# Scores and state product of a decayed linear attention in eight 64 x 32 array tiles, causal quarters only

## The chip, the cores and the metric

The kernel runs on one core of one Trainium2 chip. The metric is the device time of one execution in microseconds. TensorE (PE) multiplies, VectorE (DVE) and ScalarE (ACT) work element by element, GpSimd (POOL) does a little arithmetic on single columns, and SyncE (SP) issues the transfers.

## The reference, cut to what matters

```python
# q, k, v, f_logit: (4, 8, 768, 48)
f = 1.0 / (1.0 + np.exp(-f_logit))
for t in range(S):
    state = f[:, :, t, :, None] * state + np.einsum('bhd,bhe->bhde', k[:, :, t], v[:, :, t])
    y[:, :, t] = np.einsum('bhd,bhde->bhe', q[:, :, t], state)
# y as rows (3072, 384); RMS norm with weights rms_g; d_ff 1536
x = (silu(xn @ w_gate) * (xn @ w_val)) @ w_out
# d_ff 2048; g is 0 below -1, h above 1, (h + 1)^2 / 4 between
y = g(x @ w_in) @ w_out
```

## The kernel before, in words

The sequence is cut into chunks of C = 128 positions; there are 24 (six for each of four batches), three to a tile of N = 384 rows, so NT = 8 tiles. The heads lie in pairs: NP = 4 pairs p, and the heads r = 0, 1 of a pair occupy partitions 0 to 47 and 64 to 111 (HP = 64, D = 48). For a chunk, VectorE makes two cumulative products of the decays by scans (`after`, and `qd` by way of L721), the decayed keys `kd` and queries `qd`, and the decayed state `decayed`. TensorE then

- turns kd into kdT by four transposes (turn_kd, L300), which ScalarE copies out of the accumulator ta;
- multiplies keys by queries (score, L314): for each pair one matmul of head 0 into bank tb and one of head 1 into bank ta, each of 64 rows by 128 columns of the array with 128 moving columns. VectorE multiplies both by the 0/1 matrix `causal` (mask_scores, L752), which clears the keys that come after a query;
- computes the state's update k^T v (update, L324) into tb, which VectorE adds to `decayed` (update_state, L763);
- makes y (attend) in y_ps: for each pair the decayed state times qd in four tiles of 112 rows by 32 columns, for both heads at once (L338, 96 moving columns, of which the part between different heads is zero in `state`), and then scores times v for each head in four tiles of 128 by 32 (L344, 48 moving columns);
- turns the normalised rows (turn_x, L352), which become the input x of the projections, split in a high and a low part.

The plain float32 operands make each of these matmuls two passes in the trace. The projections of the two MLPs (L403, L425, L429, L467, L479, L483) run over the split high and low operands with 384 moving columns.

The order is written out by hand. Chunks 0 to 2 are made ahead of everything (first_attention), with matmuls between that only keep the array busy (L375). Then tile i goes through 12 steps j of the first MLP while the attention of tile i + 1 is put between the projections: 36 slots, three to a step, and chunk c of the tile is offset by 10 slots (WINDOW). On TensorE slot 4 is turn_kd, 6 score, 9 update and attend, 13 turn_x; each engine has its own list for the same slots. TensorE, VectorE and ScalarE run tiles 1 to 6 in a hardware loop (Fori). Tile 7 has no attention beside it. The second MLP follows.

Waits are semaphores that count chunks. y_made rises twice a chunk, after each half of the pairs; it frees v_sb, qd, kd and decayed. turn_kd writes into ta as soon as the masks of the chunk before are done. normalise (L769) reads y_ps when POOL has made rstd (L286, L289), and raises xs_ready. When decays are too small a general path after the main block repeats everything; it doesn't run with these inputs.

Of the kernel before, what the change touches and what calls it, by code (L numbers as in the profile page):

```python
# [17 lines left out]
F32 = mybir.dt.float32  # L18
# [40 lines left out]
def build(nc, qkf, v, rms_g, wb, wc, out, y_rows):  # L59
    ctx = ExitStack()  # L60
    with ctx:
# [29 lines left out]
        state = sb("state", [P, 2, NP, 2 * D])  # L91
        decayed = sb("decayed", [P, NP, 2 * D])
# [14 lines left out]
        causal = sb("causal", [P, C])  # L107
# [11 lines left out]
        y_ps = bank("y_ps")  # L119
        ta = bank("ta")  # L120
        tb = bank("tb")

# [80 lines left out]
        with nc.Block() as block:  # L203
# [3 lines left out]
            def _(sp):  # L207
# [23 lines left out]
                for n in range(1, CT):  # L231
                    sp.wait_ge(y_made, 2 * n)
                    load_v(n)
                    load_wb(n + 1)
# [5 lines left out]
                sp.wait_ge(y_made, 2 * CT)  # L240
# [6 lines left out]
                sp.wait_ge(y_made, 2 * CT + 2)  # L247
                load_v(CT + 1)
                load_wb(11)
                with sp.Fori(CT + 2, NCH) as n:  # L250
                    sp.wait_ge(qd_ready, n)
                    load_raw(n)
                    sp.wait_ge(y_made, n * 2)
                    load_v(n)
                stages = len(wc_stages)
                sp.wait_ge(qd_ready, NCH)
                for j in range(JC):
                    if j == 2:
                        sp.wait_ge(y_made, 2 * NCH)
# [14 lines left out]
            def _(pool):  # L274
                nc.gpsimd.memset(minus_half[:, :], -0.5).then_inc(consts_ready, 1)
                nc.gpsimd.memset(eps_col[:, :], EPS).then_inc(consts_ready, 1)
                nc.gpsimd.memset(causal[:, :], 1.0).then_inc(consts_ready, 1)
                nc.gpsimd.memset(ident[:, :], 0.0).then_inc(consts_ready, 1)
                pool.wait_ge(consts_ready, 4)
                nc.gpsimd.affine_select(out=causal[:, :], in_=causal[:, :], compare_op=ALU.is_ge, fill=0.0,  # L280
                                        base=0, pattern=[[1, C]], channel_multiplier=-1).then_inc(consts_ready, 1)
# [12 lines left out]
            def _(pe):  # L294
                def turn_kd(n, c):
                    pe.wait_ge(kd_ready, n + 1)
                    if not isinstance(n, int) or n > 0:
# [5 lines left out]
                def score(n, c, first=False):  # L303
# [7 lines left out]
                    for p in range(NP):  # L311
                        for r, t in enumerate((tb, ta)):
                            rows = slice(r * HP, (r + 1) * HP)
                            mm = pe.matmul(t[:, p * C:(p + 1) * C], kd[rows, c % 2, p, :], qd[rows, c % 2, p, :],  # L314
                                           start=True, stop=True)
                    mm.then_inc(scores_made, 1)

                def update(n):
# [3 lines left out]
                    for p in range(NP):  # L322
                        for r in range(2):
                            mm = pe.matmul(tb[r * HP:r * HP + D, p * D:(p + 1) * D], kdT[:, p, r * HP:r * HP + D],  # L324
                                           v_sb[:, r, p, :], start=True, stop=True)
                    mm.then_inc(update_made, 1)

                def attend(n, c, half):
                    if half == 0:
                        pe.wait_ge(scores_ready, n * 2 + 2)  # L330
                        pe.wait_ge(decayed_ready, n + 1)
                        if not isinstance(n, int) or n > 0:
                            pe.wait_ge(xs_ready, n)
                    for p in range(half * NP // 2, (half + 1) * NP // 2):
                        o = p * 2 * D
                        for s in range(C // QW):
                            q = slice(s * QW, (s + 1) * QW)
                            pe.matmul(y_ps[q, o:o + 2 * D], qd[0:PR, c % 2, p, q], decayed[0:PR, p, :],  # L338
                                      start=True, stop=False, skip_group_check=True)
# [15 lines left out]
                def attention(i, slot):  # L355

                    for c in range(CT):
# [884 lines left out]
```

## Time and profile before

| | us |
|---|---|
| median of 3 runs | 984.48 (984.31 to 984.51) |
| profiled execution | 984.23 |
| its span | 982.5 |
| PE matmuls busy | 966.8 (8227 records) |
| DVE busy | 585.9 (1196) |
| ACT busy | 341.8 (624) |
| POOL busy | 22.4 (58) |

The span runs from the first to the last instruction. Matmuls are pipelined: the duration of one is its latency, and the distance from one start to the next is what it costs. "PEld" is the loading of a matmul's stationary operand. Columns "128*32 128x48" are the part of the array (rows * columns) and the moving operand.

### The profile page before, as it was taken

How to read it: one execution, taken by the hardware profiler on the slowest of the kernel's cores; microseconds unless marked ns; L12 is line 12 of the kernel's file. 1: busy time of each engine (PE TensorE's matmuls, PEld its weight loads, DVE VectorE, ACT ScalarE, POOL GpSimd, SP SyncE). 2: the span in 40 equal slices, each digit the busy share in tenths (PEclk: the TensorE clock that was granted, in tenths of full speed). 3: DMA queues.
4: the chain of work that ended last, by engine and by line, in shares of the span. 5: the costliest groups of instructions: out<-in, count | busy, mean ns of one | idle time of the engine just before them, and what ended most of it. 6: DMA issues, size and time to landing. Idle time of an engine off the chain costs nothing.

```text
span 982.5 us, 20662 instructions
## 1 busy us (share of the span) xinstructions
PE 966.8 (98%) x8227; PEld 943.4 (96%) x8227; DVE 585.9 (60%) x1196; ACT 341.8 (35%) x624; POOL 22.4 (2%) x58
## 2 busy tenths in 40 slices
PE   6899999999999999999999999999999999999998
PEld 6899999999999999999999999999999999999998
DVE  8778665574674765665565565555545554545454
ACT  2343322322322222223224454344344344434433
POOL 0100000000000000000000000000000000000000
PEclk9999999999999999999999999999999999999999
DMA  5541111011120110111120400000000000000000
GB/s 194 190 149 43 40 42 50 32 48 40 40 71 9 61 52 13 68 40 40 40 87 17 136 27 1 25 0 24 0 24 0 24 0 19 5 5 19 0 25 25
DMA packets 15774, 42.32 MB, mean 43 GB/s; under 512 B 1408, under 2 KB 8064, under 8 KB 15744
## 3 DMA queue, kind: packets, MB, share of 16 engines
q1 hardware_dynamic: 15744, 41.88, 12.5%
q8 instruction: 23, 0.38, 0.2%
q14 instruction: 7, 0.06, 0.0%
HBM read 37.16 MB, written 4.72 MB: 43 GB/s over the span
## 4 chain that ended last, share of the span: by engine, by line
PE 95%; DVE 3%; issue 1%; POOL 0%; ACT 0%; DMA 0%; DVEq 0%; POOLq 0%
PE gate_ps L403 15%; PE val_ps L403 15%; PE acc L479 13%; PE gate_ps L467 10%; PE val_ps L467 10%; PE acc L425 10%; PE acc L483 7%; PE acc L429 5%; PE tb L314 2%; PE y_ps L338 2%; PE y_ps L344 2%; PE tb L324 1%; DVE qd L721 1%; PE ta L300 1%; DVE after L700 1%
## 5 line engine op out<-in xcount | busy, mean ns | idle before, releaser
L837 DVE TENSOR_TENSOR h_lo<-h_buf,h_hi 128x384 fp32r<-128x384 f32 x224 | 123.3, 551 | 13.2 <-ACT h_hi L648 6.2
L641 ACT ACTIVATE act_buf<-act_buf,half_col 128x384 f32<-128x384 f32 x128 | 78.8, 615 | 140.5 <-DVE act_buf L887 140.5
L479 PE MATMUL acc<-h_hi,w_hi 128*128 128x384 f32 x381 | 127.5, 335 | 0.0
L479 PE MATMUL acc<-h_hi,w_lo 128*128 128x384 f32 x381 | 127.4, 334 | 0.0
L584 ACT ACTIVATE act_buf<-gate_ps 128x384 f32<-128x384 f32 x96 | 47.2, 492 | 177.1 <-PE gate_ps L403 177.1
L589 ACT ACTIVATE h_hi<-h_buf 128x384 fp32r<-128x384 f32 x96 | 50.5, 526 | 167.6 <-DVE h_buf L832 167.6
L403 PE MATMUL gate_ps<-x_hi,w_hi 128*128 (+1 forms) x288 | 99.2, 344 | 1.0 <-issue 0.6
L425 PE MATMUL acc<-h_hi,w_hi 128*128 128x384 f32 x288 | 99.1, 344 | 0.0
L403 PE MATMUL val_ps<-x_hi,w_hi 128*128 (+1 forms) x288 | 99.1, 344 | 0.0
L403 PE MATMUL gate_ps<-x_hi,w_lo 128*128 (+1 forms) x288 | 96.5, 335 | 0.0
L403 PE MATMUL val_ps<-x_hi,w_lo 128*128 (+1 forms) x288 | 96.4, 335 | 0.0
L403 PE MATMUL gate_ps<-x_lo,w_hi 128*128 (+1 forms) x288 | 96.4, 335 | 0.0
L425 PE MATMUL acc<-h_hi,w_lo 128*128 128x384 f32 x288 | 96.4, 335 | 0.0
L403 PE MATMUL val_ps<-x_lo,w_hi 128*128 (+1 forms) x288 | 96.4, 335 | 0.0
L648 ACT ACTIVATE h_hi<-h_buf 128x384 fp32r<-128x384 f32 x128 | 67.2, 525 | 80.4 <-DVE h_buf L892 80.4
L483 PE MATMUL acc<-h_lo,w_hi 128*128 128x384 f32 x381 | 86.5, 334 | 0.0
L826 DVE TENSOR_TENSOR h_buf<-gate_ps,act_buf 128x384 f32<-128x384 f32 x96 | 53.1, 553 | 52.6 <-ACT act_buf L584 52.2
L832 DVE TENSOR_TENSOR h_buf<-val_ps,h_buf 128x384 f32<-128x384 f32 x96 | 53.5, 557 | 38.0 <-PE val_ps L403 36.2
L887 DVE TENSOR_SCALAR act_buf<-val_ps 128x384 f32<-128x384 f32 x64 | 35.6, 557 | 67.0 <-PE val_ps L467 67.0
L479 PEld LDWEIGHTS acc<-h_hi,w_hi 128*128 128x128 f32 x381 | 71.5, 188 | 0.6
L479 PEld LDWEIGHTS acc<-h_hi,w_lo 128*128 128x128 f32 x381 | 71.5, 188 | 0.0
L887 DVE TENSOR_SCALAR act_buf<-gate_ps 128x384 f32<-128x384 f32 x64 | 35.5, 555 | 55.3 <-PE gate_ps L467 55.3
(117 smaller groups left out, 1989.3 us busy)
## 6 DMA issues: line engine op xcount, KB each, us to landing
raw<-qkf_dram SPq DMA_DIRECT2D x21, 768.0 KB, 4.3
x<-wb_dram SPq DMA_DIRECT2D x12, 576.0 KB, 5.2
v_sb<-v_dram SPq DMA_DIRECT2D x24, 192.0 KB, 2.8
out_dram<-x SPq DMA_DIRECT2D x7, 576.0 KB, 2.8
raw<-wc_dram SPq DMA_DIRECT2D x7, 384.0 KB, 3.1
x<-qkf_dram SPq DMA_DIRECT2D x2, 768.0 KB, 6.8
kd<-wc_dram SPq DMA_DIRECT2D x3, 384.0 KB, 3.1
qd<-wc_dram SPq DMA_DIRECT2D x3, 384.0 KB, 3.9
```

Source lines behind the costliest of these rows:

```text
L403: mm = pe.matmul(bank[:, 0:N], wb_part(w, j, part, k), x[:, par, k, :], start=(k == 0 and x is x_hi and w is w_hi), stop=(k == KM - 1 and ...
L425: pe.matmul(acc[:, m, 0:N], wb_part(w, j, 2, m), h_hi[:, j % 2, :], start=(j == 0 and w is w_hi), stop=False)
L467: mm = pe.matmul(t[:, 0:N], wc_part(w, j, 0, k), x[:, i % 2, k, :], start=(k == 0 and x is x_hi and w is w_hi), stop=(k == KM - 1 and w is ...
L479: pe.matmul(acc[:, m, 0:N], wc_part(w, j, 1, m), h_hi[:, j % 2, :], start=(j == 0 and w is w_hi), stop=False)
L483: mm = pe.matmul(acc[:, m, 0:N], wc_part(w_hi, j, 1, m), h_lo[:, j % 2, :], start=False, stop=(j == JC - 1))
L589: nc.scalar.activation(h_hi[:, j % 2, :], h_buf[:, j % 2, :], ACT.Copy).then_inc(h_hi_ready, 1)
L641: nc.scalar.activation(act_buf[:, j % 2, :], act_buf[:, j % 2, :], ACT.Square, bias=half_col[:, :], scale=0.5).then_inc(square_ready, 1)
L648: nc.scalar.activation(h_hi[:, j % 2, :], h_buf[:, j % 2, :], ACT.Copy)\
L826: nc.vector.tensor_tensor(h_buf[:, j % 2, :], gate_ps[:, 0:N], act_buf[:, 0, :], ALU.mult)\
L832: nc.vector.tensor_tensor(h_buf[:, j % 2, :], val_ps[:, 0:N], h_buf[:, j % 2, :], ALU.mult)\
L837: nc.vector.tensor_tensor(h_lo[:, j % 2, :], h_buf[:, j % 2, :], h_hi[:, j % 2, :].bitcast(F32), ALU.subtract).then_inc(done, 1)
L887: nc.vector.tensor_scalar(act_buf[:, j % 2, :], t[:, 0:N], 1.0, -1.0, ALU.min, ALU.max)\
```

## The change

The score product is cut into quarters of 32 keys (QW). A quarter s of an even pair is multiplied only by the queries from 32 s on, so with 128, 96, 64 and 32 columns. In odd pairs the order of the four key quarters is reversed in kd, in v and in the mask, so their quarters have 32, 64, 96 and 128 columns. With the two heads that makes eight tiles of 64 rows by 32 columns. The three chunks of the opening use all 128 columns for every quarter. The product of the decayed state (recall) gets the same eight tiles, one head at a time with 48 columns, and stands ahead of update. y has a bank for each head, the second one shared with ta (in the opening: banks 1 and 2 of acc); columns of y, weights and rms_g are ordered by head parity. State and decayed lose their zero blocks. Update is cut at row 32 into two tiles for each head. turn_kd waits for xs_ready. y_made rises once a chunk. kd is made by two instructions. POOL makes the second mask. The loops over tiles 1 to 6 become straight code on TensorE, ScalarE and VectorE.

```diff
-        state = sb("state", [P, 2, NP, 2 * D])
-        decayed = sb("decayed", [P, NP, 2 * D])
+        state = sb("state", [P, 2, NP, D])
+        decayed = sb("decayed", [P, NP, D])
-        causal = sb("causal", [P, C])
+        causal = sb("causal", [P, 2, C])
-        y_ps = bank("y_ps")
-        ta = bank("ta")
+        y_ps = ctx.enter_context(nc.psum_tensor("y_ps", [P, 2, 512], F32))
         tb = bank("tb")
+        ta = y_ps[:, 1, :]
+        y_first = acc[:, 1:3, :]
...
+                for s in range(C // QW):
+                    rows = slice(s * QW, (s + 1) * QW)
+                    pool.wait_ge(consts_ready, 6 + s)
+                    nc.gpsimd.affine_select(out=causal[rows, 1, :], in_=causal[rows, 1, :], compare_op=ALU.is_ge,
+                                            fill=0.0, base=s * QW + QW - C, pattern=[[1, C]],
+                                            channel_multiplier=-1).then_inc(consts_ready, 1)
...
                 def turn_kd(n, c):
                     pe.wait_ge(kd_ready, n + 1)
-                    if not isinstance(n, int) or n > 0:
+                    if not isinstance(n, int) or n >= CT:
+                        pe.wait_ge(xs_ready, n)
+                    elif n > 0:
                         pe.wait_ge(scores_ready, 2 * n)
...
                     for p in range(NP):
-                        for r, t in enumerate((tb, ta)):
-                            rows = slice(r * HP, (r + 1) * HP)
-                            mm = pe.matmul(t[:, p * C:(p + 1) * C], kd[rows, c % 2, p, :], qd[rows, c % 2, p, :],
-                                           start=True, stop=True)
+                        for s in range(C // QW):
+                            t0 = 0 if first else C - (s + 1) * QW if p % 2 else s * QW
+                            for r, t in enumerate((tb, ta)):
+                                rows = slice(r * HP, (r + 1) * HP)
+                                mm = pe.matmul(t[s * QW:(s + 1) * QW, p * C + t0:(p + 1) * C],
+                                               kd[rows, c % 2, p, s * QW:(s + 1) * QW],
+                                               qd[rows, c % 2, p, t0:C], start=True, stop=True)
                     mm.then_inc(scores_made, 1)
+
+                def recall(n, c, y):
+                    pe.wait_ge(scores_ready, n * 2 + 2)
+                    pe.wait_ge(decayed_ready, n + 1)
+                    if not isinstance(n, int) or n > 0:
+                        pe.wait_ge(xs_ready, n)
+                    for p in range(NP):
+                        for s in range(C // QW):
+                            q = slice(s * QW, (s + 1) * QW)
+                            for r in range(2):
+                                rows = slice(r * HP, (r + 1) * HP)
+                                pe.matmul(y[q, r, p * D:(p + 1) * D], qd[rows, c % 2, p, q], decayed[rows, p, :],
+                                          start=(p == 0), stop=False, skip_group_check=True)
...
-                            mm = pe.matmul(tb[r * HP:r * HP + D, p * D:(p + 1) * D], kdT[:, p, r * HP:r * HP + D],
-                                           v_sb[:, r, p, :], start=True, stop=True)
+                            for d0, d1 in ((0, QW), (QW, D)):
+                                rows = slice(r * HP + d0, r * HP + d1)
+                                mm = pe.matmul(tb[rows, p * D:(p + 1) * D], kdT[:, p, rows],
+                                               v_sb[:, r, p, :], start=True, stop=True)
...
-                def attend(n, c, half):
...
+                def attend(n, y):
+                    for p in range(NP):
                         for r in range(2):
-                            h = slice(o + r * D, o + (r + 1) * D)
                             for s in range(C // QW):
                                 q = slice(s * QW, (s + 1) * QW)
-                                mm = pe.matmul(y_ps[q, h], scores[:, r, p, q], v_sb[:, r, p, :],
+                                mm = pe.matmul(y[q, r, p * D:(p + 1) * D], scores[:, r, p, q], v_sb[:, r, p, :],
                                                start=False, stop=True, skip_group_check=True)
...
                         elif o == 9:
+                            recall(n, c, y_ps)
                             update(n)
-                            attend(n, c, 0)
-                            attend(n, c, 1)
+                            attend(n, y_ps)
...
                     for n in range(CT):
+                        recall(n, n, y_first)
                         update(n)
-                        attend(n, n, 0)
+                        attend(n, y_first)
                         if n + 1 < CT:
                             turn_kd(n + 1, n + 1)
-                        attend(n, n, 1)
-                        if n + 1 < CT:
                             score(n + 1, n + 1, True)
...
-                with pe.Fori(1, NT - 1) as i:
+                for i in range(1, NT - 1):
                     gated_mlp(i, i + 1)
...
-                    nc.vector.tensor_tensor(kd[:, c % 2, :, :], raw[:, 1, :, :], after[:, :, :], ALU.mult)\
-                        .then_inc(kd_ready, 1)
+                    nc.vector.tensor_tensor(kd[:, c % 2, 0::2, :], raw[:, 1, 0::2, :], after[:, 0::2, :], ALU.mult)
+                    turned, k_odd, after_odd = (x.rearrange("d a (s t) -> d a s t", s=C // QW) for x in
+                                                (kd[:, c % 2, 1::2, :], raw[:, 1, 1::2, :], after[:, 1::2, :]))
+                    nc.vector.tensor_tensor(turned[:, :, ::-1, :], k_odd, after_odd, ALU.mult).then_inc(kd_ready, 1)
```

The loops of ScalarE and VectorE change as TensorE's does. The masks, the square sum and the normalisation read the new layouts with as many elements as before. v is turned on the host as well, and the general path gets a copy of v that isn't (`v_rows`).

## Rows read from the trace of the kernel before

**Rows 1.** Page, part 1: busy time, share of the span, instructions of each engine.
```profile
PE 966.8 (98%) x8227; PEld 943.4 (96%) x8227; DVE 585.9 (60%) x1196; ACT 341.8 (35%) x624; POOL 22.4 (2%) x58
```

**Rows 2.** Stretches: length, busy time of each engine, granted clock, DMA share, GB/s.
```profile
0.00:40.00 40.00, 29.72 (x520) 27.25 (x521) 30.89 (x74) 12.29 (x22) 5.60 (x16) 1.00 0.63 223
40.00:100.00 60.00, 58.33 (x663) 54.73 (x662) 48.35 (x94) 24.36 (x42) 2.25 (x6) 1.00 0.26 90
280.00:340.00 60.00, 60.00 (x669) 57.72 (x668) 36.69 (x85) 16.76 (x36) 2.43 (x6) 1.00 0.11 36
```

**Rows 3.** TensorE's waits: us in total, times, longest.
```profile
PE acc L429 <- DVE h_lo L837: 1.3, 2, 0.8
```

**Rows 4.** Timeline of a score product: start, us, engine, line, operation.
```profile
324.55 0.33 PE L403 MATMUL gate_ps<-x_lo,w_hi 128*128 x1
324.72 0.34 PE L403 MATMUL gate_ps<-x_hi,w_lo 128*128 x1
324.99 0.37 PE L314 MATMUL tb<-qd,kd 64*128 64x128 f32 x1
325.00 0.37 PE L314 MATMUL ta<-qd,kd 64*128 64x128 f32 x1
325.20 0.27 PE L314 MATMUL tb<-qd,kd 64*128 64x128 f32 x1
...
325.87 0.27 PE L314 MATMUL tb<-qd,kd 64*128 64x128 f32 x1
325.88 0.27 PE L314 MATMUL ta<-qd,kd 64*128 64x128 f32 x1
326.08 0.45 PE L403 MATMUL val_ps<-x_hi,w_hi 128*128 x1
```

**Rows 5.** Timeline of update and attend in slot 9.
```profile
301.53 0.56 PE L324 MATMUL tb<-v_sb,kdT 128*48 128x48 f32 x16
302.02 0.37 PE L338 MATMUL y_ps<-decayed,qd 112*32 112x96 f32 x8
302.21 0.36 PE L344 MATMUL y_ps<-v_sb,scores 128*32 128x48 f32 x16
302.39 0.35 PE L338 MATMUL y_ps<-decayed,qd 112*32 112x96 f32 x8
302.56 0.35 PE L344 MATMUL y_ps<-v_sb,scores 128*32 128x48 f32 x16
...
303.52 0.44 PE L403 MATMUL gate_ps<-x_hi,w_hi 128*128 x1
```

**Rows 6.** Timeline of the weight loads of one group.
```profile
302.02 0.16 PEld L338 LDWEIGHTS y_ps<-decayed,qd 112*32 112x32 f32 x8
```

**Rows 7.** Timeline of VectorE in the opening.
```profile
13.53 0.55 DVE L746 TENSOR_TENSOR decayed<-state,whole 128x384 f32<-128x384 f32 x1
13.99 0.69 DVE L730 TENSOR_TENSOR kd<-x,after 128x512 f32<-128x512 f32 x1
14.60 0.72 DVE L763 TENSOR_TENSOR state<-tb,decayed 48x192 f32<-48x192 f32 x2
```

**Rows 8.** Timeline of the engines around a tile's first turn_kd.
```profile
322.08 0.55 DVE L837 TENSOR_TENSOR h_lo<-h_buf,h_hi 128x384 fp32r<-128x384 f32 x1
322.42 0.34 PE L425 MATMUL acc<-h_hi,w_lo 128*128 128x384 f32 x1
322.69 0.45 PE L429 MATMUL acc<-h_lo,w_hi 128*128 128x384 f32 x1
```

**Rows 9.** The chain that ended last, in the opening: start, us, what.
```profile
23.00 0.53 PE ta L300 x4
```

**Rows 10.** DMA queues: 0 to 100 us (first row) and 166 to 520 us (others).
```profile
q8 instruction: 9, 0.15, 0.6%
...
DMA packets 6816, 15.93 MB, mean 45 GB/s; under 512 B 544, under 2 KB 4384, under 8 KB 6816
q1 hardware_dynamic: 6816, 15.93, 13.7%
```

More of the change, by code:

```diff
@@ L56, with build @@
 SMALLEST = 2.0 ** -60
-def build(nc, qkf, v, rms_g, wb, wc, out, y_rows):
+def build(nc, qkf, v, v_rows, rms_g, wb, wc, out, y_rows):
     ctx = ExitStack()
@@ L231, in _ @@
                 for n in range(1, CT):
-                    sp.wait_ge(y_made, 2 * n)
+                    sp.wait_ge(y_made, n)
                     load_v(n)
@@ L239, in _ @@
                     load_wb(j)
-                sp.wait_ge(y_made, 2 * CT)
+                sp.wait_ge(y_made, CT)
                 load_v(CT)
@@ L246, in _ @@
                 load_wb(10)
-                sp.wait_ge(y_made, 2 * CT + 2)
+                sp.wait_ge(y_made, CT + 1)
                 load_v(CT + 1)
@@ L252, in _ @@
                     load_raw(n)
-                    sp.wait_ge(y_made, n * 2)
+                    sp.wait_ge(y_made, n)
                     load_v(n)
@@ L258, in _ @@
                     if j == 2:
-                        sp.wait_ge(y_made, 2 * NCH)
+                        sp.wait_ge(y_made, NCH)
                     if j >= stages:
@@ L374, in keep_warm @@
                     for _ in range(count):
-                        pe.matmul(acc[:, 0, 0:P], ident[:, :], causal[:, :], start=True, stop=True)
+                        pe.matmul(acc[:, 0, 0:P], ident[:, :], causal[:, 0, :], start=True, stop=True)
                 def first_attention():
@@ L682, in _ @@
                 gated_mlp(0, 1, split=True)
-                with act.Fori(1, NT - 1) as i:
+                for i in range(1, NT - 1):
                     gated_mlp(i, i + 1)
@@ L740, in decay_state @@
                     if not isinstance(n, int) or n > 0:
-                        dve.wait_ge(y_made, n * 2)
+                        dve.wait_ge(y_made, n)
                     if c > 0:
@@ L761, in update_state, with normalise @@
                     for r in range(2):
-                        rows, cols = slice(r * HP, r * HP + D), slice(r * D, (r + 1) * D)
-                        ins = nc.vector.tensor_tensor(state[rows, 1, :, cols], u[rows, :, :],
-                                                      decayed[rows, :, cols], ALU.add)
+                        rows = slice(r * HP, r * HP + D)
+                        ins = nc.vector.tensor_tensor(state[rows, 1, :, :], u[rows, :, :],
+                                                      decayed[rows, :, :], ALU.add)
                     ins.then_inc(state_ready, 1)
-                def normalise(n):
+                def normalise(n, y=y_ps):
                     dve.wait_ge(rstd_ready, n + 1)
-                    nc.vector.scalar_tensor_tensor(out=xs[:, :], in0=y_ps[:, 0:DM], scalar=rstd[:, :],
-                                                   in1=g_rows[:, :], op0=ALU.mult, op1=ALU.mult)\
+                    heads = [x[:, :].rearrange("t (r m) -> t r m", r=2) for x in (xs, g_rows)]
+                    nc.vector.scalar_tensor_tensor(out=heads[0], in0=y[:, :, 0:NP * D], scalar=rstd[:, :],
+                                                   in1=heads[1], op0=ALU.mult, op1=ALU.mult)\
                         .then_inc(xs_ready, 1)
@@ L935, in _ @@
                         dve.wait_ge(g_loaded, 16)
-                    normalise(n)
+                    normalise(n, y_first)
                 rest_x(0, CT - 1, (gate_ps, val_ps)[(CT - 1) % 2])
                 gated_mlp(0, 1, split=True)
-                with dve.Fori(1, NT - 1) as i:
+                for i in range(1, NT - 1):
                     gated_mlp(i, i + 1)
```

58 lines of the change are left out of this document (26 added, 32 removed).

## The prediction

> **What bounds the kernel now.** I read four views in this order. The engine shares [rows 1] have TensorE's matmuls busy for 966.8 of 982.5 us and no other engine above 60%. The table of stretches [rows 2] shows where most of the other 16 us are: 10.3 in the first 40 us, 1.7 in the next 60, none in a stretch of the middle; the granted clock is 1.00 in all three, the 2.4 GHz level. The list of TensorE's waits [rows 3] holds single waits of the opening and two of 1.3 us in all on h_lo. So from 40 us on the time is the sum of what TensorE is given, and whatever shortens its stream shortens the kernel one for one, until another engine falls behind. The timelines of one score product [rows 4] and of one slot of update and attend [rows 5] are then the price list. A chunk is scored and attended 24 times, 3 times in the opening, where other engines set the pace, and 21 times between projections, where TensorE does. The profiled execution took 984.23 us, 1.7 us outside its span; the median of the runs is 984.48, 0.25 above it, so a saving counted in the profile is taken from either.
>
> **What a pass costs.** Each float32 matmul stands in the trace as two passes: a chunk has 8 score matmuls and [rows 4] are from its 16 passes, eight steps of one pass for each accumulator. A step is 0.11 us for 128 columns, and both 64-row tiles start within 0.01 us and run beside each other. In [rows 5] a group of L344 is 16 passes of 48 columns in 0.17 us on four column tiles, four steps of 0.042; a group of L338 is 8 passes of 96 columns in 0.17, two steps of 0.084. So a pass costs 0.875 ns a column and tiles that differ run side by side. How fast passes can be issued: the eight weight loads of L338 cover 0.16 us while one takes 0.11 [rows 6], so they start within 0.05, some 7 ns apart. Passing between tilings costs: last L403 to first L314 is 0.27 where projections follow each other at 0.17, so 0.10 more; 0.09 on the way out (325.88 to 326.08, less 0.11 of its own); the same between L324 and L338.
>
> **Scores, after.** Eight tiles of 64 x 32 take 64 passes, of 128, 96, 64 and 32 columns for the quarters of an even head pair and the other way round for an odd one. Each tile gets 160 columns over two head pairs, in two passes, twice: 640 columns, 0.56 us. With 0.03 for the first weights and 0.05 until the eighth tile has started it is 0.64; 64 starts at 7 ns are 0.45 and fit beneath. Before, the product takes 0.89 from first to last start and 0.11 more: 1.00 [rows 4]. Saved: 0.36 a chunk. Bounds: if passes must start in program order, a tile with a long pass holds up all behind it. The even pair's first passes start at 0 and its second ones from 0.11 on; the odd pair's first passes come from 0.22, its quarter of 128 columns at 0.26, the second pass of that at 0.37, and only beside it the next even pair. So two head pairs take 0.37, four with the last pass and the first weights 0.88, and 0.12 is saved. If the two row halves don't overlap it is 1.12 + 0.05, 0.17 more than now. Ways in and out are as before. I take 0.36: in [rows 4] ta's first pass starts 0.01 us after tb's and does not wait for the second pass of tb's matmul, which the kernel issues ahead of it. The three products of the opening keep all 128 columns and gain nothing.
>
> **The state product (recall), update, attend.** Now L324 starts at 301.53 and the next projection at 303.52 [rows 5]; less 0.09 for the way out that is 1.90. After: recall has 64 passes of 48 columns over eight tiles, eight steps. A step's columns need 0.042, its eight starts 8 x 7 = 0.055, so starts bind: 0.44, with the first weights and the last pass 0.50. Bounds: 0.37 if columns bind; if starts are no denser than the mean of an L344 group (0.17 / 16 = 10.6 ns), 0.70. I take 0.50, nearest to the dense starts of [rows 6]. The 32 passes of L338 cost 4 x 0.17 = 0.68 now. Then one change of tiling, 0.10, that also stands there now. Update has twice the instructions, in four tiles instead of two: eight steps of 0.042 and 0.03 for the first, 0.36, against 0.39 up to the last end. Attend has the same 64 passes in one run: 16 steps of 0.042, 0.68. Sum 0.50 + 0.10 + 0.36 + 0.68 = 1.64; saved 0.26 a chunk (0.06 to 0.39).
>
> A rule speaks against all this. [Rows 5] have L344's matmuls starting 10.6 ns apart. The Trainium skill (TensorE: Matmul & The Clock Gate, section on the warm-up mystery) says that start to start never drops below about 25 ns however few the columns. By that page of the Trainium skill, an estimate: 64 x 25 ns is 1.6 us for scores and as much for recall, 0.6 and 0.9 more than now, 31 us over 21 chunks, near 1016. The trace disagrees for differing tiles, so this rule gets no chance.
>
> **Other engines.** VectorE's kd product becomes two of 256 columns. Back to back, 512 columns take 0.61 from start to start (13.99 to 14.60), 384 take 0.46 [rows 7]: about 0.06 fixed and 1.05 ns a column, so the split costs 0.06. Decayed falls from 384 to 192 columns, 0.20 less. Both normally lie beside TensorE's stream. The exception is the first chunk of a tile: h_lo is made at 322.08 to 322.63 behind that chain and L429 starts at 322.69, 0.27 after the one before it instead of 0.17 [rows 8]. There the 0.06 lands on the path: 7 tiles, 0.4 us. Decayed comes later than that and gives nothing back. The mask, the state sum, the square sum and the normalisation keep their element counts. turn_kd waits for xs of the chunk before, since ta now shares its accumulator; queued behind it are the projections. VectorE issues that normalise just ahead of the kd product which turn_kd already waits for, so the wait is never the last to end: nothing. POOL's four selections lie at 2 to 4 us, the masks that need them are made just before 13.53 [rows 7]. SP's waits on y_made count by one and stay in place; y_made rises once instead of twice, at the same end. The longer program of the three engines is a rival below.
>
> **Opening.** Recall stands ahead of update, so update_state, now free at 14.60 [rows 7], waits for decayed (13.53 + 0.35), 0.60 of recall and the change, and 0.36 of update: 14.84, with two hand-overs about 15.0, 0.4 late, of which 0.2 comes back from the shorter decayed. In the other two chunks recall waits for both masks: again 0.4 each for VectorE. Against that y is whole 0.26 earlier, and 0.5 more since turn_kd (0.53 in the middle of attend [rows 9]) moves behind it; that is what normalise waits for only where VectorE isn't late. Bounds +1.2 and -1.0 over all; I take +0.3. In the first tile TensorE is waiting for VectorE's h_lo (1.3 us [rows 3]), so part of the 3 x 0.62 saved there returns as waiting: +0.6 of at most 1.9.
>
> **Sum.** 21 x (0.36 + 0.26) = 13.0 saved, 0.4 + 0.3 + 0.6 = 1.3 given back: 11.7. From 984.23 that is 972.5, from the median 972.8; I say 972.8.
>
> **The rivals.**
> Starts in program order. Then scores save only 0.12: 21 x 0.38 = 8.0, less 1.3 is 6.7, so 977.8. For it: every pass in the trace has as many columns as its neighbours on other tiles, so no row shows a short one overtaking. Against it: second passes of four tiles come after all four first ones, as tiles with queues of their own would do. The Trainium skill (TensorE: Matmul & The Clock Gate, section on packing small matmuls) says that matmuls start and end in strict program order; by it this rival is the result, and no row here shows which holds for unequal widths. Chance 0.25.
> Dispatch binds. 10.6 ns a start makes recall 0.70 and scores 0.73: 21 x (0.27 + 0.06) - 1.3 = 5.6 saved, 978.8. For it: no row shows more than eight dense starts in succession. Chance 0.12.
> Only four tiles run at once. Recall 16 x 0.042 + 0.03 = 0.70, scores 1.17: 21 x (0.17 - 0.06) + 1.3 = 3.6 slower, 988. Two row tiles and four column tiles each overlap in the trace, the product of both isn't shown. Chance 0.04.
> Instructions don't arrive. The loops over six tiles become straight code, so each tile's instructions must be fetched. In the first 100 us, straight code too, nine packets of 16 KB came, each taking some 1.07 us (0.6% of 16 engines x 100 us, by nine); from 166 to 520 us, in the loop, none [rows 10]. TensorE issued 2 x 1183 loads and matmuls in these [rows 2], 263 a packet. A chunk will need 4 + 64 + 64 + 32 + 64 + 3 = 231 pairs of load and matmul, 1.8 packets, most in bursts of 0.6 and 1.6 us. If each packet is waited for in full, 1.9 us x 21 = 40 is lost and the time is 1012; the sign turns at 0.56 us a chunk. Against it: the opening already runs 135 pairs a chunk in straight code and its waits all name another cause [rows 3]; nine packets of 256 instructions each for 2362 issued show fetching that keeps pace through that code. Chance 0.07.
> Beyond these, 0.52 for the forecast; within it, or better if recall's starts are denser, 0.1 lies below 971.
>
> **How the numbers follow.** No change that a measurement can tell is 0.2%, 2 us: 982.5 to 986.5. Forecast, ordered starts and bound dispatch are all faster: 0.89. Fetches that cost about what is gained give 0.03 for the same; four tiles at once (0.04) and fetches that cost more (0.04) make slower 0.08. For 8 in 10: the low end by recall at 0.37 and an opening at its best, 972.8 - 2.7 - 0.6, is 969.5; the high end takes in both smaller savings, 979.5.
>
> **What would show it.** In a later tile, first to last start of the score product 0.6 us (0.8 if ordered, with short passes of the next head pair waiting), recall 0.45, L403 coming 1.0 us after the last one before scores and 2.0 after the last L429; TensorE's matmul records up by 96 a chunk, 2300, with its busy time about 11 us lower; new waits on h_lo no more than a microsecond. Wrong would be gaps on TensorE put down to issue, or a recall of 0.7.

## The result: 2.2% slower, where 1.2% faster was forecast

The changed kernel takes 1006.76 us (1004.63 to 1008.38, four runs) against 984.50 for the kernel before beside it: ratio 1.0222 (95% interval 1.0202 to 1.0243). The forecast was 972.8, range 969.5 to 979.5. The profiled execution took 1006.56, its span is 1004.9.

First the busy times and the instruction queue, from the page of the changed kernel:

```profile
PE 973.8 (97%) x10531; PEld 944.8 (94%) x10531; DVE 582.5 (58%) x1220; ACT 341.0 (34%) x624; POOL 22.5 (2%) x62
q8 instruction: 70, 1.15, 0.5%
```

2304 more matmul records than in [rows 1], 96 a chunk as expected, but 7 us more busy time instead of 11 less. The second row is the queue over which instructions are fetched (packets, MB, share). Of it [rows 10] show nine packets in 100 us and none in the loop; now 70 come over the whole run, where the page of the kernel before has

```profile
q8 instruction: 23, 0.38, 0.2%
```

The same windows as in [rows 2], and two stretches of the opening (start:end, length, then for each engine busy us and records, the granted clock, DMA share, GB/s):

```profile
0.00:40.00 40.00, 26.91 (x762) 24.06 (x763) 27.22 (x69) 10.47 (x19) 4.94 (x18) 0.87 0.56 196
40.00:100.00 60.00, 56.90 (x795) 53.26 (x795) 45.97 (x96) 22.94 (x41) 2.24 (x6) 0.97 0.32 106
280.00:340.00 60.00, 57.43 (x772) 55.08 (x759) 34.54 (x81) 15.16 (x33) 2.43 (x6) 0.97 0.13 38
14.00:29.00 15.00, 12.02 (x412) 10.81 (x413) 9.06 (x26) 2.56 (x5) 0.90 (x2) 0.66 0.20 57
29.00:44.00 15.00, 10.86 (x274) 9.87 (x272) 9.09 (x14) 4.68 (x9) 2.38 (x4) 0.89 0.80 271
```

The first 40 us hold 2.8 us less of matmul time, at a granted clock of 0.87 instead of 1.00, and the middle, gapless before, now loses 2.6 of 60. What for is in the list of TensorE's waits (engine, accumulator and line, releaser, total us, times, longest):

```profile
PE acc L360 <- issue: 5.2, 2, 3.3
PE y_ps L360 <- issue: 5.2, 3, 2.0
PE gate_ps L418 <- DVE h_buf L845: 4.7, 7, 1.3
...
PE val_ps L418 <- issue: 1.7, 1, 1.7
```

Two sorts are new: waits on nothing but issue (the engine stands, and the profile shows nothing that it waits for) in the middle of attend (L360), and seven waits of a gate projection for h_buf.

One score product, timeline of TensorE (start, us, engine, line, operation, tile and moving operand; of the first group the rows of tb alone):

```profile
456.12 0.29 PE L325 MATMUL tb<-qd,kd 64*32 64x128 f32 x1
456.13 0.27 PE L325 MATMUL tb<-qd,kd 64*32 64x96 f32 x1
456.16 0.21 PE L325 MATMUL tb<-qd,kd 64*32 64x32 f32 x1
456.21 0.19 PE L325 MATMUL tb<-qd,kd 64*32 64x32 f32 x1
456.23 0.22 PE L325 MATMUL tb<-qd,kd 64*32 64x64 f32 x1
456.25 0.27 PE L325 MATMUL tb<-qd,kd 64*32 64x128 f32 x1
...
456.56 0.29 PE L325 MATMUL y_ps<-qd,kd 64*32 64x128 f32 x1
456.58 0.26 PE L325 MATMUL tb<-qd,kd 64*32 64x96 f32 x1
456.59 0.26 PE L325 MATMUL y_ps<-qd,kd 64*32 64x96 f32 x1
456.61 0.24 PE L325 MATMUL tb<-qd,kd 64*32 64x64 f32 x1
456.63 0.24 PE L325 MATMUL y_ps<-qd,kd 64*32 64x64 f32 x1
456.64 0.21 PE L325 MATMUL tb<-qd,kd 64*32 64x32 f32 x1
456.66 0.21 PE L325 MATMUL y_ps<-qd,kd 64*32 64x32 f32 x1
...
456.92 0.27 PE L325 MATMUL y_ps<-qd,kd 64*32 64x128 f32 x1
```

At first the passes start 7 ns apart (eight of them from 456.12 to 456.17), and second passes of 32 columns (.21) start before those of 128 (.25), which the kernel issues ahead of them: tiles start out of program order. In the next head pair the kernel issues its 32 columns first and its 128 last, and they start the other way round: the second row of 128 on tb is at .25, the next of 32 not before .36. From .56 on the pace is another: seven matmuls in 0.10 us, one per 17 ns, while each has two passes and the tiles stand free. First to last start is 0.80 us, against 0.89 in [rows 4] and 0.6 forecast.

A slot 9 late in the run and one with a break:

```profile
462.01 0.81 PE L340 MATMUL y_ps<-decayed,qd 64*32 64x48 f32 x64
462.74 0.54 PE L351 MATMUL tb<-v_sb,kdT 128*32 128x48 f32 x32
463.10 0.86 PE L360 MATMUL y_ps<-v_sb,scores 128*32 128x48 f32 x64
463.89 0.44 PE L418 MATMUL gate_ps<-x_hi,w_hi 128*128 128x384 f32 x1
...
278.44 0.81 PE L340 MATMUL y_ps<-decayed,qd 64*32 64x48 f32 x64
279.18 0.54 PE L351 MATMUL tb<-v_sb,kdT 128*32 128x48 f32 x32
279.53 0.81 PE L360 MATMUL y_ps<-v_sb,scores 128*32 128x48 f32 x57
282.33 0.29 PE L360 MATMUL y_ps<-v_sb,scores 128*32 128x48 f32 x7 [1.99 <-issue]
```

The undisturbed slot takes 1.88 from start to next projection, against 1.99 in [rows 5]: recall with the change of tiling 0.73 (0.60 forecast), update 0.36, attend with the way out 0.79, both about as forecast. In the other, TensorE has started 57 of attend's 64 passes and then starts none for 2 us.

**Where the time went.** I compared each block between projections in TensorE's stream (its cost is the distance from the projection before to the one after, less one projection's own 0.174) in both traces:

| | us |
|---|---|
| score product, 21 x (1.186 to 1.096) | -1.9 |
| slot 9 undisturbed, 21 x (2.081 to 1.980) | -2.1 |
| breaks in slot 9 at 174.0, 205.5, 247.3, 278.2, 322.1, 351.6 | +8.3 |
| turn_x of the tile's first chunk, behind it a gate that waits for h_buf, 7 tiles | +5.7 |
| h_lo after the first chunk, 6 tiles at 0.33 instead of 0.27 | +0.4 |
| a break between two projections at 106.1 | +1.0 |
| ten starts 0.32 apart after the break at 282, instead of 0.17 (granted clock 0.53 from 282.3 to 285.9, so nearly all at the 1.2 GHz level, where the 4 us before the slot have 1.00) | +1.7 |
| turn_kd, the first tile and h_lo's rest | +0.4 |
| opening: first projection at 44.55 instead of 35.61 | +8.9 |
| sum | +22.4 |

Between the last matmuls of the two traces (1000.82 and 978.45) lie 22.4.

### The profile page after: what moved, and what is told of

The parts are those of the page before. It is cut to its first block, busy times and chain, and to the rows that moved or that the text cites. A ratio compares the mean times of both kernels' runs of the same rounds, so it can differ in the third digit from the quotient of the medians.

```text
span 1004.9 us, 24802 instructions
## 1 busy us (share of the span) xinstructions
PE 973.8 (97%) x10531; PEld 944.8 (94%) x10531; DVE 582.5 (58%) x1220; ACT 341.0 (34%) x624; POOL 22.5 (2%) x62
## 3 DMA queue, kind: packets, MB, share of 16 engines
q8 instruction: 70, 1.15, 0.5%
## 4 chain that ended last, share of the span: by engine, by line
PE 89%; DVE 5%; issue 3%; POOL 1%; ACT 1%; DMA 0%; POOLq 0%; DVEq 0%; ACTq 0%
PE gate_ps L418 14%; PE val_ps L418 14%; PE acc L494 13%; PE gate_ps L482 10%; PE val_ps L482 10%; PE acc L440 8%; PE acc L498 7%; PE acc L444 4%; PE tb L325 2%; DVE qd L736 2%; PE y_ps L340 2%; PE tb L351 1%; PE y_ps L360 1%; PE y_ps L309 1%; PE acc L391 1%
## 5 line engine op out<-in xcount | busy, mean ns | idle before, releaser
L418 PE MATMUL gate_ps<-x_hi,w_hi 128*128 128x384 f32 x288 | 99.2, 344 | 5.1 <-DVE h_buf L845 4.7
L418 PE MATMUL val_ps<-x_hi,w_hi 128*128 128x384 f32 x288 | 99.6, 346 | 1.7 <-issue 1.7
L418 PE MATMUL gate_ps<-x_lo,w_hi 128*128 128x384 f32 x288 | 96.5, 335 | 0.8 <-issue 0.8
L418 PE MATMUL val_ps<-x_hi,w_lo 128*128 128x384 f32 x288 | 97.0, 337 | 0.0
L418 PE MATMUL val_ps<-x_lo,w_hi 128*128 128x384 f32 x288 | 97.0, 337 | 0.0
L418 PE MATMUL gate_ps<-x_hi,w_lo 128*128 128x384 f32 x288 | 96.5, 335 | 0.0
L498 PEld LDWEIGHTS acc<-h_lo,w_hi 128*128 128x128 f32 x381 | 67.9, 188 | 0.0
```

The lines of the kernel that those rows point to most:

```text
L418: mm = pe.matmul(bank[:, 0:N], wb_part(w, j, part, k), x[:, par, k, :], start=(k == 0 and x is x_hi and w is w_hi), stop=(k == KM - 1 and ...
L498: mm = pe.matmul(acc[:, m, 0:N], wc_part(w_hi, j, 1, m), h_lo[:, j % 2, :], start=False, stop=(j == JC - 1))
```

## The experiments

**Loops and straight code.** e2 is the kernel before with its loops over tiles written out; e1 is the changed kernel with the loops put back:

```diff
-                with pe.Fori(1, NT - 1) as i:        # e2; e1 the other way; ACT and DVE alike
+                for i in range(1, NT - 1):
                     gated_mlp(i, i + 1)
```

In e1 a semaphore step of TensorE's sequencer also stands between two register waits and the first matmul of score and of recall.

> The kernel before with only the three loops over tiles 1 to 6 turned into straight code. Theory A: packets rise from 23 to some 55, but a chunk has 135 matmul passes instead of 231 and fetching keeps up as it does in its opening: 984 to 986. A stronger form of A (any straight code of this rate breaks now and then): 988 to 993 with waits on issue in attend. Rival B: 984.5.

> The changed kernel with tiles 1 to 6 in hardware loops again on TensorE, ScalarE and VectorE; the waits ahead of score and recall are carried by a semaphore step of TensorE's sequencer. Theory A (instructions fetched from memory arrive too late for bursts of short matmuls): the breaks inside attend at 205, 251, 282, 322 and 352 us go (1.8 + 1.5 + 2.2 + 0.2 + 0.4 us) and with them the 3.4 us at the 1.2 GHz clock level after the fourth (1.8), so some 8 us less: 999, about 27 fetched packets instead of 70, no waits on issue in the middle; the opening keeps its breaks. Rival B (the breaks come from the tiles' own queues or from transfers of data): they stay, 1006 to 1007. If the longer loop body no longer stays in the instruction store, packets stay at 70 and the time at 1006 or above.

e2: 984.57, ratio 1.000 (0.999 to 1.001). It fetches 52 packets instead of 23, and every block costs what it costs before. e1: 1015.16, ratio 1.0319 (1.0302 to 1.0336), slower than the change itself. From e2's page, then e1's page and waits:

```profile
q8 instruction: 52, 0.85, 0.3%
```

```profile
q8 instruction: 79, 1.29, 0.5%
PE val_ps L423 <- issue: 16.0, 11, 1.8
PE gate_ps L423 <- DVE h_buf L850: 4.2, 7, 1.3
```

So straight code by itself costs nothing at 135 pairs of load and matmul a chunk, and the loop doesn't rescue the change: its body has grown from 1514 TensorE instructions a round in the trace (729 matmuls and as many loads among them) to 2096, and it is fetched anew each time round (ten packets from 250 to 323 us, one round). The forecast's rival had the cause (instructions that don't arrive) but not the condition.

**The size of the loop.** e5 is the kernel before, loops kept, with nothing but update in four tiles:

```diff
-                            mm = pe.matmul(tb[r * HP:r * HP + D, p * D:(p + 1) * D], kdT[:, p, r * HP:r * HP + D],
+                            for d0, d1 in ((0, QW), (QW, D)):
+                                rows = slice(r * HP + d0, r * HP + d1)
+                                mm = pe.matmul(tb[rows, p * D:(p + 1) * D], kdT[:, p, rows],
```

> The kernel before with one edit: update is cut at row 32 into tiles of 128 x 32, the tiling of attend, so that no change of tiling lies between them. Theory E (of the 0.10 us that the changed kernel saves in slot 9 all comes from one change of tiling less, none from recall's eight tiles): slot 9 costs 1.98 instead of 2.08, 21 x 0.10 = 2.1 less, 982.4. Rival: the gap between L324 and L338 was the wait for decayed and the masks: it stays, 984.5.

994.74, ratio 1.0107 (1.0091 to 1.0124). Slot 9 falls from 2.081 to 1.926, and yet the kernel loses 10 us:

```profile
q8 instruction: 69, 1.13, 0.5%
PE val_ps L405 <- issue: 9.1, 5, 2.1
```

Five waits, at 177.7, 248.4, 319.1, 389.9 and 462.4, one for each return of the loop, of about 2 us. One round of it, 250.4 to 321.1, in a window of that length:

```profile
250.40:321.10 70.70, 68.97 (x777) 66.13 (x777) 42.89 (x96) 19.19 (x40) 2.44 (x6) 1.00 0.14 44
```

777 pairs of load and matmul, and 1610 instructions with those of the sequencer. At 729 and 1514 the trace of before has no packet from the second round on [rows 10]; at 1610 this round alone has nine. A saving of 0.155 a chunk cost 2 a tile.

The 0.155 says something of the change too. Its whole slot 9 saves 0.101, and four-tile update in the old order saves more than that by itself: from its start to that of the matmuls behind it 0.35 instead of 0.49, with no change of tiling left between. So recall in eight tiles, which was to save 0.18, saved nothing: with the change of tiling that follows it takes 0.73, where the passes of L338 took 0.68.

**The order of update.** e3 is the changed kernel with update ahead of recall, e4 the same in loops:

```diff
-                            recall(n, c, y_ps)
                             update(n)
+                            recall(n, c, y_ps)
```

> The changed kernel with update ahead of recall, still straight code. Theory C (update made 0.75 us later holds VectorE's queue, so h, the square sum, the normalisation and the next chunk's scans come later, and gate(8) waits for h_buf 0.81 us a tile): the seven waits of gate_ps on h_buf (4.7 us in all, 5.7 against the kernel before) go, one more change of tiling costs 0.10 x 21 = 2.1, the opening gets some 1 us back: about 1002 to 1003. Rival D (the split kd product or the second waits of turn_kd make gate(8) late): the waits stay and the time rises to 1009.

> Both edits together. If A and C are separate the gains add: 999 less 4 to 5, about 994 to 995. What is left over 984.5 is then the opening with its breaks and its time at the lower clock (about 9 us), less some 2 us that the shorter products of later chunks save. Under B and D: 1006 or more.

e3: 1002.12, ratio 1.0183 (1.0166 to 1.02); its trace is of the fastest of four runs, 998.91. The blocks of turn_x fall from 11.54 to 5.84 us in all, before had 5.80, and of the h_buf waits (4.7, seven) this is left in e3's list:

```profile
PE gate_ps L418 <- DVE h_buf L845: 0.4, 1, 0.4
```

Slot 9 rises to 2.118, since update now wants a change of tiling on either side; 21 x 0.14 = 2.9 of the 5.7 go back. The first projection comes at 42.35, 2.2 earlier. The chain can be followed in the changed kernel, VectorE, ScalarE and GpSimd, behind a slot 9 that starts at 153.79:

```profile
155.14 0.72 DVE L781 TENSOR_TENSOR state<-tb,decayed 48x192 f32<-48x192 f32 x2 [4.37 <-PE tb L351]
155.89 0.56 DVE L845 TENSOR_TENSOR h_buf<-gate_ps,act_buf 128x384 f32<-128x384 f32 x1
156.49 0.56 DVE L851 TENSOR_TENSOR h_buf<-val_ps,h_buf 128x384 f32<-128x384 f32 x1
...
159.21 0.62 DVE L788 SCALAR_TENSOR_TENSOR xs<-y_ps,rstd,g_rows 128x384 f32<-128x384 f32 x1 [0.45 <-POOL rstd L296]
...
160.90 1.61 DVE L736 TENSOR_TENSOR_SCAN qd<-raw,inv_whole 128x128 f32<-128x128 f32 x4
162.43 0.53 DVE L845 TENSOR_TENSOR h_buf<-gate_ps,act_buf 128x384 f32<-128x384 f32 x1
```

```profile
157.08 0.53 ACT L604 ACTIVATE h_hi<-h_buf 128x384 fp32r<-128x384 f32 x1 [3.73 <-DVE h_buf L851]
157.51 0.47 ACT L564 ACTIVATE xs<-y_ps 128x384 f32<-128x384 f32 x1
```

The next gate waits in TensorE's stream for the h_buf product at 162.43, which frees gate_ps:

```profile
163.10 0.41 PE L418 MATMUL gate_ps<-x_hi,w_hi 128*128 128x384 f32 x1 [0.57 <-DVE h_buf L845]
```

VectorE works through its list in order. The state sum (L781) stands in it ahead of both h_buf products, and it can't start before update. With recall first it starts 1.35 after slot 9 does; in e3 0.62 after (151.24 and 151.86). All behind it slides, by way of ScalarE's square sum and GpSimd's rstd, to the next h_buf product at 162.43.

e4: 1017.17, ratio 1.034 (1.0323 to 1.0357), again 79 packets. The 5.7 of turn_x are gone here too, and the time still isn't below e1's: slot 9 takes 2.8 more in all (58.23 against 55.43), which is the further change of tiling, and the first projection comes 2.6 later (43.36 against 40.75). What its 21 slots take beyond the undisturbed cost is the same in both, 13.8 and 13.9. So the totals of the looped versions don't show the order's gain; the waits and blocks of e3 do.

**The score product cut in halves, and the recall left alone.** e6 is the kernel before in straight code with two key halves of 64 a head instead of four quarters, the second half with 64 queries only, and kd, v and mask reversed by halves in odd pairs: four tiles of 64 x 64. e7 adds e5's update:

```diff
-                        for r, t in enumerate((tb, ta)):
...
-                            mm = pe.matmul(t[:, p * C:(p + 1) * C], kd[rows, c % 2, p, :], qd[rows, c % 2, p, :],
+                        for s in range(1 if first else C // KW):        # KW = 64
+                            keys = slice(0, C) if first else slice(s * KW, (s + 1) * KW)
+                            t0 = 0 if first else C - (s + 1) * KW if p % 2 else s * KW
+                            for r, t in enumerate((tb, ta)):
...
+                                mm = pe.matmul(t[keys, p * C + t0:(p + 1) * C], kd[rows, c % 2, p, keys],
+                                               qd[rows, c % 2, p, t0:C],
...
```

> The kernel before as straight code, with the score product cut in halves of 64 keys instead of quarters (four tiles of 64 x 64, 128 and 64 queries, reversed in odd pairs; the opening keeps its two tiles). Theory F (the quarters' product is limited by the supply of instructions: 16 matmuls stand ready in TensorE's queue, after that one comes every 17 ns and the first of them 0.3 us late; 32 matmuls exceed the queue, the 16 of the halves don't): columns bind, 4 x 192 x 0.875 = 0.67 us and 0.06 around, 0.73 instead of 1.00; score costs 0.92 instead of 1.19 (quarters: 1.10). 21 x 0.27 - 0.4 for the split kd product = 5.3 less, 979.2. Rival G (unequal widths in one tile group cost what they save): 1.1 again, 983.

> Both edits. A chunk has 167 pairs of load and matmul, between the 135 of before and the 231 of the changed kernel. E and F together: 977.1. If the supply from memory already fails at 167, waits on issue of 1 to 2 us show in attend and the time is 980 or more.

e6: 980.26, ratio 0.9955 (0.9943 to 0.9968), the score block 0.925. e7: 978.13, ratio 0.9935 (0.9922 to 0.9948), the fastest of all and faster than both kernels; slot 9 costs 1.921. Its windows have no gap in the middle:

```profile
280.00:340.00 60.00, 60.00 (x680) 57.92 (x669) 39.54 (x93) 17.36 (x37) 2.43 (x6) 1.00 0.14 45
```

Halves leave each of four tiles 768 columns (0.67 us) where quarters leave each of eight 640 (0.56), but they need 16 matmuls instead of 32, and the measured block is 0.17 shorter. So the columns don't bind the quarters; the number of matmuls fits. The tiles' width differs as well between the two, and no run holds it fixed.

**Quarters in that version, and quarters without the triangle.** e12 is e7 with the quarters of the change (KW = 32); e10 is the kernel before in straight code with quarters that keep all 128 queries:

```diff
-KW = 64
+KW = 32
```

> The best kernel so far (978.1: scores in halves, update in four tiles, the old recall in tiles of 112 x 32, straight code) with scores in quarters: also 199 pairs a chunk, of which 64 in the score product. Theory F: score 1.10 instead of 0.92, so 981.8 if no burst breaks; theory A allows breaks on issue of some us more, since the bursts are denser than at 167 pairs.

> The kernel before as straight code (984.5), with each score product of the 21 later chunks cut in quarters of 32 keys but over all 128 queries: no column less, 64 passes instead of 16, 183 pairs of load and matmul a chunk. Theory A and F: columns still bind (8 x 0.11 and 0.15 around), score costs 1.1 to 1.3, time 985 to 989 from it; if fetching fails at 183 pairs, breaks on issue of 1 to 2 us are added, 990 or more. Rival G: no breaks, and the time follows the columns alone, 984.5.

e12: 981.05, ratio 0.997 (0.9958 to 0.9983); the score block is back at 1.095, and 21 x 0.17 = 3.6 of e7's gain with it (2.9 measured). e10: 984.81, ratio 0.9999 (0.999 to 1.0009): eight tiles with 1024 columns each cost 1.18, as two tiles do before. So all eight do run side by side, and the rival of four tiles falls. Of the 1.18, 0.90 are the columns; cutting them to 640 (0.56) gives 1.095 and not 0.84, so another bound comes out, and by e7 and e12 it goes with the number of matmuls. e10 and e12 issue 183 and 199 pairs a chunk in straight code, in bursts of at most 112 and 128, and no slot 9 of theirs has a break. A window of 200 us in e12:

```profile
160.00:360.00 200.00, 200.00 (x2674) 191.41 (x2673) 125.79 (x291) 56.22 (x119) 7.31 (x18) 1.00 0.13 43
```

**The length of the burst, and where it falls.** e11 is e3 with halves for quarters, so it has e12's 199 pairs a chunk, but 160 of them in one burst in slot 9, where e12 has 128. e9 is e3 with 16 more of the matmuls that keep the array busy in the opening, which moves all that follows by 64 instructions:

```diff
-WARM_START, WARM_SCORES, WARM_ROWS, WARM_LAST = 10, 6, 3, 8
+WARM_START, WARM_SCORES, WARM_ROWS, WARM_LAST = 10, 6, 3, 24
```

> The changed kernel with update ahead of recall (1002.1) and its scores in halves instead of quarters, everywhere: 199 pairs a chunk instead of 231. Theory F: score 0.92 instead of 1.10, 3.7 us less. Theory A: fewer breaks in the middle and in the opening; together 985 to 995. If breaks don't depend on the number of instructions: 998.4.

> The changed kernel with update ahead of recall (1002.1; breaks on issue in slot 9 at 171, 202, 243, 274, 316 and 346 us) and 16 more matmuls that only keep the array busy, in the opening, where TensorE waits for the last rows anyway; they shift all that follows by 64 instructions against the 256 of a fetched packet. Theory A (a burst breaks when the request for the next packet falls at its start): the six breaks of 1.4 to 2.3 us move to other chunks or change in number, the opening's stay; 995 to 1010, and which of it can't be told ahead. Rival B (they hang on the loads of qkf, v or weights): they stay in the same six chunks, 1002.

e11: 995.00, ratio 1.0097 (1.007 to 1.0123). Four slots are broken, by 2.1, 0.9, 0.8 and 1.8 us, at 236.9, 289.5, 339.4 and 498.8. With e12's count of instructions a chunk and breaks like e3's, it is the burst and not the sum that runs dry. e9: 996.77, ratio 1.012 (1.0091 to 1.0149). Its first projection is 3.3 later than e3's, and the six breaks of e3 between 170 and 346 are gone; one slot breaks, at 498.9, where e3's does not; two more pauses, at 62 and 433, are of 0.2 us or less. The same 200 us in e3 and in e9, a fence each:

```profile
160.00:360.00 200.00, 193.78 (x2764) 184.06 (x2763) 117.58 (x273) 54.26 (x113) 6.34 (x16) 1.00 0.14 45
```

```profile
160.00:360.00 200.00, 200.00 (x2864) 190.57 (x2863) 122.07 (x282) 55.61 (x116) 6.37 (x16) 1.00 0.14 45
```

The same instructions in the same order, 6.2 us apart, by where they stand in the program.

The traces show where. From e2 to the changed kernel there are 2 x 2304 more loads and matmuls and 18 more packets, 256 instructions each. Number TensorE's records (loads, matmuls, sequencer) by their starts up to a slot 9 and count two a pair within it, and each of the 23 broken slots of the changed kernel, e3, e8, e9 and e11 stops at a number that leaves 190 when divided by 256, the same place of a packet. That place lies behind the 142nd to 160th pair of the burst in all 23. In the other 82 slots of these traces it never lies there; where it lies behind the 128th to 139th they run through. In the changed kernel and in e3 it is pair 157, 160, 150, 153, 143 and 146 of the same six chunks, though these come 3 to 6 us apart in time. The pauses between two projections (106.1 in the changed kernel) stand within four records of it, 1 to 7 pairs behind a burst. So a burst of 160 pairs breaks when it has run through the last 14 pairs or more of one packet and then all 128 of the next. Bursts of 128 pairs can't do that. How long a burst must be at the least, between 128 and 160, no run tried. And e3 has none from 360 to 460 because the place falls elsewhere there.

**The opening.** e8 is e3 whose three opening score products use the two tiles of before:

```diff
-                        for s in range(C // QW):
+                        for s in range(1 if first else C // QW):
+                            keys = slice(0, C) if first else slice(s * QW, (s + 1) * QW)
...
```

> The changed kernel with update ahead of recall (1002.1) and, in the three chunks of the opening only, scores in two tiles of 64 x 128 instead of eight of 64 x 32: the same columns, 16 passes instead of 64 a chunk. Theory A: the opening's breaks on issue (4.1 us) come from that burst, and the projections start at 38 to 40 us instead of 42.4; 998 to 1000, the breaks of the middle may move. Rival B: the opening is late through VectorE and the order of its products: 42 us and 1002.

998.71, ratio 1.0149 (1.0134 to 1.0163); the first projection comes at 40.45, 1.9 before e3's. In the opening of the changed kernel:

```profile
15.38 0.44 PE L360 MATMUL acc<-v_sb,scores 128*32 128x48 f32 x24
17.78 1.03 PE L360 MATMUL acc<-v_sb,scores 128*32 128x48 f32 x40 [1.95 <-issue]
...
35.18 0.55 PE L360 MATMUL acc<-v_sb,scores 128*32 128x48 f32 x33
39.01 0.54 PE L360 MATMUL acc<-v_sb,scores 128*32 128x48 f32 x31 [3.27 <-issue]
```

Of the 8.9 us, 2.2 go in e3 and another 1.9 in e8, and of the 4.8 left e8's own list of waits puts 3.9 on one break in attend. These steps aren't clean prices of the order and of the quarters: e1 has the opening of the changed kernel and its first projection at 40.75, and e4, with update first, is 2.6 later than e1. Breaks and clock shift with each version. The 40 passes behind the first break last 1.03 where 64 last 0.86 in a later slot; it is in this stretch that the granted clock is 0.66. The breaks of e8 between 306 and 481 are not those of e3 (170 to 346), which fits e9 and the place in the packet.

## Why the prediction was wrong

Between the forecast and the result lie 34 us: 9.0 that the products didn't save, 11.0 of breaks in the steady part with the slow projections after one, 5.7 from the order of update, and 8.6 of the opening.

**The rate of a burst** (the step "how fast passes can be issued"). I read 7 ns from eight loads in succession and 10.6 from a group of L344, and used the first for 64. The rate holds only for about the first 16 matmuls, which stand ready. After that one matmul of two passes starts every 17 ns, as the changed kernel's rows at 456.6 show. Scores saved 0.09 instead of 0.36, slot 9 0.10 instead of 0.26: 4.0 us instead of 13.0. e6, e12 and e10 show the bound from three sides. The bound of 10.6 ns a start was itself not the upper one for the scores ("dispatch binds" would make their block 0.92, and 1.096 was measured), and recall with its change of tiling took 0.73 where 0.60 was forecast.

**Starts in program order**: rightly not chosen. The Trainium skill (TensorE: Matmul & The Clock Gate, section on packing small matmuls) has matmuls start in strict program order. The trace disagrees, with a short second pass at 456.21 before a long one at 456.25 that is issued ahead of it.

The same page of the Trainium skill (section on the warm-up mystery) gives some 25 ns from start to start at the least; the estimate from it was 1016. The trace disagrees for differing tiles, 7 ns in the burst and 8.3 a pass beyond it, though this and not my rate named the right quantity: a price a matmul, not a column.

**The rival of missing instructions** was costed as an average, a packet for each 256 instructions and a chance of 0.07, and set aside because the opening of before keeps pace at 135 pairs a chunk. It is not an average. e10 and e12 keep pace at 183 and 199 too. It failed where 160 pairs came in 1.9 us, in six of 21 chunks, for 8.3 us, and once more between projections: only where a packet's end fell late in the burst. I had noted that most packets would be needed "in bursts of 0.6 and 1.6 us", and priced that only as all or nothing.

**Straight code** costs nothing itself (e2), so the term at which it stood was right. That the loop of before stood within 7% of the size at which it stops being free (e5) I hadn't looked for. It was not part of this change's loss, but it decides what a part of it is worth alone.

**The order of update.** I priced the later state sum in the opening and called it hidden in the steady state, where I looked at the waits on kd and h_lo only. The in-order list behind it cost 5.7 (e3). The step that failed is "other engines": of a moved instruction I priced what waits for its result, not what stands behind it in its consumer's queue.

**The opening**: +8.9 instead of +0.3. Its bounds (+1.2 and -1.0) held neither the breaks, nor a slower clock after them, nor that eight tiles of 128 columns need four times the instructions of two where they bring nothing. How the 8.9 divide stays open.

**Right were** update in four tiles (0.36), attend (0.79 with the way out, 0.77 forecast), the split of kd (0.06 a tile), the count of records, xs and POOL's masks at nothing, and that eight tiles run at once.

## What to carry to other kernels

Price small matmuls by their number as well as by their columns, from a row with as many in succession as the change will have; cutting a product finer than that rate allows returns nothing (quarters 1.095, halves 0.925). Before a tuned loop's body grows, or a burst is lengthened, look at the instruction queue of the trace: a loop that fetches nothing may be near its limit, and a burst longer than a packet's 128 pairs can break, by its place in the program, so that an unrelated shift moves the loss. When an instruction moves, follow the list of the engine that consumes it, behind the consumer.

## What the hardware showed that I had not expected

- Instruction packets of 16 KB (1.15 MB in 70), one per 256 instructions (4608 more, 18 packets more). A burst of 160 pairs runs dry where a packet's end falls behind its 142nd to 160th pair, in 23 slots of 105, and in none otherwise. TensorE then stands for 0.1 to 2.4 us in the steady part, and for 4.0 at the longest in an opening (e9).
- A loop body of 1514 TensorE instructions goes round without a packet, one of 1610 is fetched each time (nine packets a round), with some 2 us at its top. Where between these two the limit lies was not tried.
- At 456.12 to 456.40 the 32 passes of the first 16 score matmuls start in 0.28 us, as dense as 7 ns apart; further matmuls start 17 ns apart.
- Tiles take their passes each in its own order, short ones overtaking long ones on other tiles.
- After a break of 2 us at 280 the next ten projections started 0.32 apart; after the other five they did not. Why that one alone stays open. So does why the pause is 0.1 to 0.9 us where the packet's end falls behind pair 142 to 148, and 1.3 to 2.4 beyond.
